# Attention: exponent rows transferred two units sooner, ahead of raw weights, and the row terms' constant operand made in one operation

## The reference

```python
m_new = maximum(f + m, i)
C = exp(f + m - m_new) * C + exp(i - m_new) * outer(v, k)
n = exp(f + m - m_new) * n + exp(i - m_new) * k
y = sigmoid(o) * (C @ q) / maximum(abs(n @ q), 1)
...
x = leaky_relu(x @ w_in) @ w_out                # 1536 x 320, hidden 2048
P = exp(x @ w_gate - max), eight rounds of row and column normalising
out = sum over 8 experts of P[:, e] * (relu(x @ w1[e]) @ w2[e])
```

## Time and profile before

| | |
|---|---|
| median of 3 runs | 940.11 us (940.0 to 940.24) |
| the profiled execution | 939.58 us |
| its span, first to last instruction | 937.9 us |
| PE busy | 928.4 us, 99% |
| VectorE, ScalarE, GpSimd busy | 646.0, 354.1, 436.7 us |
| TensorE clock granted | full in every slice |
| DMA | 42.39 MB, 45 GB/s over the span |

### The profile page before, as it was taken

The page is one execution under the profiler, slowest core; times in us unless marked ns, Lnnn a source line. Parts: engine busy times, 40 slices in busy tenths (PEclk is TensorE's granted clock), DMA queues, the critical chain, the costliest instruction groups (busy, mean ns, idle before and its releaser), DMA issues.

```text
span 937.9 us, 16679 instructions
## 1 busy us (share of the span) xinstructions
PE 928.4 (99%) x6508; PEld 888.6 (95%) x6518; DVE 646.0 (69%) x1071; ACT 354.1 (38%) x671; POOL 436.7 (47%) x489
## 2 busy tenths in 40 slices
PE   9999999999999999999999999999999999999998
PEld 6999888888799999999999999999999999999998
DVE  7877555467778989876666666666666666667665
ACT  6674534344444233233332432333243233323221
POOL 4462311076598645656633651663365166336000
PEclk9999999999999999999999999999999999999999
DMA  7990321011011111021101111111111111110000
GB/s 124 216 146 2 93 64 34 1 35 34 0 38 32 35 35 56 14 59 43 53 17 35 56 47 35 35 38 31 35 50 53 35 35 34 35 35 1 30 28 29
DMA packets 82796, 42.39 MB, mean 45 GB/s; under 512 B 54270, under 2 KB 82302, under 8 KB 82718
## 3 DMA queue, kind: packets, MB, share of 16 engines
q1 hardware_dynamic: 82542, 41.23, 17.2%
q10 hardware_dynamic: 176, 0.10, 0.0%
HBM read 39.13 MB, written 2.11 MB: 44 GB/s over the span
## 4 chain that ended last, share of the span: by engine, by line
PE 88%; DVE 6%; SPq 3%; issue 1%; ACT 1%; DMA 1%; POOL 0%; DVEq 0%; POOLq 0%; ACTq 0%
PE psB L1720 12%; PE psB L1721 11%; PE psB L1722 11%; PE psA L1706 8%; PE psA L1705 8%; PE psA L1704 8%; PE psA L1703 8%; PE psA L1633 8%; PE psB L1652 2%; PE psB L1653 2%; PE psB L1654 2%; PE psA L1513 1%; PE psB L1536 1%; DVE gl L1431 1%; DMA rhs<-parts_d 1%
## 5 line engine op out<-in xcount | busy, mean ns | idle before, releaser
L693 POOL TENSOR_TENSOR wst<-raw_w,wst 128x128 fp32r<-128x128 f32 (+2 forms) x192 | 163.1, 862 | 303.7 <-ACT wst L920 174.9
L1720 PE MATMUL psB<-w2s,gh 128*128 128x320 f32 x768 | 238.6, 311 | 0.9 <-DVE acc L1405 0.9
L1722 PE MATMUL psB<-w2s,gl 128*128 128x320 f32 x768 | 237.3, 309 | 0.0
L1721 PE MATMUL psB<-w2s,gh 128*128 128x320 f32 x768 | 237.3, 309 | 0.0
L1431 DVE SCALAR_TENSOR_TENSOR gl<-part,gh 128x512 fp32r<-128x512 f32 x192 | 160.4, 875 | 63.4 <-ACT gh L1035 62.8
L1035 ACT ACTIVATE gh<-part 128x512 fp32r<-128x512 f32 x192 | 110.7, 624 | 245.2 <-DVE part L1425 245.1
L1705 PE MATMUL psA<-xop,wst 128*128 128x256 f32 x672 | 190.2, 283 | 0.0
L1706 PE MATMUL psA<-xop,wst 96*128 96x256 f32 x672 | 190.2, 283 | 0.0
L1704 PE MATMUL psA<-xop,wst 128*128 128x256 f32 x672 | 190.2, 283 | 0.0
L1703 PE MATMUL psA<-xop,wst 128*128 128x256 f32 x672 | 190.0, 283 | 0.0
L1720 PEld LDWEIGHTS psB<-w2s,gh 128*128 128x128 f32 x768 | 144.6, 188 | 1.4 <-DVE gl L1431 1.1
(11 more groups left out here) (204 smaller groups left out, 1376.8 us busy)
## 6 DMA issues: line engine op xcount, KB each, us to landing
raw_w<-in_moe_w_dram SPq DMA_DIRECT2D x32, 320.0 KB, 3.2
raw_w<-in_moe_w_dram SPq DMA_DIRECT2D x32, 256.0 KB, 2.6
raw_w<-in_moe_w_dram SPq DMA_DIRECT2D x96, 64.0 KB, 2.5
qs<-in_q_dram SPq DMA_DIRECT2D x12, 160.0 KB, 3.4
ks<-in_k_dram SPq DMA_DIRECT2D x12, 160.0 KB, 3.7
vz<-in_v_dram SPq DMA_DIRECT2D x12, 160.0 KB, 4.1
og<-in_o_gate_dram SPq DMA_DIRECT2D x12, 160.0 KB, 4.1
out_dram<-acc SPq DMA_DIRECT2D x5, 320.0 KB, 2.5
```

The source lines that it names most:

```text
L693: return pool.tensor_tensor(dst, raw, high.bitcast(F32), ALU.subtract)
L1720: pe.matmul(bank, gh[:, slot, cols], w2[:, f, 0, :], start=first, stop=False)
L1721: pe.matmul(bank, gh[:, slot, cols], w2[:, f, 1, :], start=False, stop=False)
L1722: last = pe.matmul(bank, gl[:, slot, cols], w2[:, f, 0, :], start=False, stop=end)
```

## The change

Three edits. SyncE: the rows of units 4 and 5 are issued before the output gates and the first raw weights, and inside the loop each step n issues the rows of unit n + 2 behind its own q, k and v. GpSimd: only slot 0 is padded before `cut_row` and `lhs`. VectorE: the eight operations of `fill` become one `tensor_tensor` with both inputs broadcast.

```diff
             load_v(2)
+            for b in range(B):
+                sp.wait_ge(x_done, b + 1)
+                chunk_rows(sp, 2, b)
             load_gates_out(0, range(B, U_IT))
+            load_v(3)
             first_w1(0)
-            load_v(3)
             first_w2(0)
-            for c in range(2, NC):
-
-                for b in range(B):
-                    n = B * c + b
-                    sp.wait_ge(x_done, n - 2 * B + 1)
-                    chunk_rows(sp, c, b)
-                    load_qk(n)
...
+            for n in range(2 * B, NU):
+                load_qk(n)
...
+                load_v(n)
+                if n + B < NU:
+                    sp.wait_ge(x_done, n - B + 1)
+                    chunk_rows(sp, (n + B) // B, n % B)
...
-            for j in range(U_IT):
-                slot_pads(j).then_inc(pads, 1)
+            slot_pads(0).then_inc(pads, 1)
             pool.memset(cut_row[:], 0.0).then_inc(consts, 1)
...
                 pool.tensor_copy(lhs[s][:], cut_row[:].unsqueeze(1).to_broadcast([P, B, L])).then_inc(lhs_ok, 1)
+            for j in range(1, U_IT):
+                slot_pads(j).then_inc(pads, 1)
...
-            fill(0, 0).then_inc(fill_ok, 1)
+            dve.tensor_tensor(rhs[0][:, 0, :, :], at_row[:].unsqueeze(1).to_broadcast([P, H, L]),
+                              head_rows[:].unsqueeze(2).to_broadcast([P, H, L]), ALU.add).then_inc(fill_ok, 1)
```

More of the change, by code:

```diff
@@ L544, in _ @@
             load_v(2)
+            for b in range(B):
+                sp.wait_ge(x_done, b + 1)
+                chunk_rows(sp, 2, b)
             load_gates_out(0, range(B, U_IT))
+            load_v(3)
             first_w1(0)
-            load_v(3)
             first_w2(0)
-            for c in range(2, NC):
-                for b in range(B):
-                    n = B * c + b
-                    sp.wait_ge(x_done, n - 2 * B + 1)
-                    chunk_rows(sp, c, b)
-                    load_qk(n)
[L556 to L566, removed]
+            for n in range(2 * B, NU):
+                load_qk(n)
+                if n == U_IT:
+                    load_gates_out(1)
+                if n == 2 * U_IT - 1:
+                    load_gates_out(2)
+                load_v(n)
+                if n + B < NU:
+                    sp.wait_ge(x_done, n - B + 1)
+                    chunk_rows(sp, (n + B) // B, n % B)
+                if n == U_IT + 1:
+                    first_w1(1)
+                if n == U_IT + 2:
+                    first_w2(1)
+                if n == U_IT + 3:
+                    first_w1(KT)
             for a in range(KT):
```

## The result

The changed kernel takes 942.63 us in the median of 13 executions (941.8 to 947.86); the kernel before, beside it, 940.22 (938.59 to 941.31, 13). The ratio of the two is 1.0047 [1.0034, 1.006]. It is slower, and the median lies 1.4 us above my range. The executions of after fall into two groups: seven between 941.8 and 942.63, with a mean granted clock of 1.0 (0.998 in the profiled one), and six between 945.64 and 947.86, with 0.994 to 0.996. There are two losses to explain: some 2 to 3 us in every execution (2.8 between the profiled ones), and 3 to 6 more in half of them. The profiled execution (942.4 us, span 940.7) is of the first group; its span is 2.8 longer than before's 937.9.

The account below looks back on a forecast made before the run. PE, busy 99% of the span, was taken as the bound. Removing 2.03 us of row waits, mostly offset by later q and k, gave -0.3 us against 940.11: forecast 939.8 us, range 938.4 to 941.2.

Parts of the forecast that it names:

- The rows: PE's waits for row loads at the exponents of units 4 and 8 both go, 2.03 us.
- the sum: PE's arrivals and k waits at units 4, 5, 8; the end moves by s - 1.03, not below -2.03 us.
- Unit 8: At its transposes the 0.70 us row wait goes, k lands at 58.47, PE waits 0.79; 0.13 us is left.
- s: Delay of each q and k load in SyncE's queue behind one more pair of rows: taken as 0.9 us.
- The bound of 2.4 for s: Upper end of the q and k delay: two row pairs issued near 20 us with nothing behind making it up.
- The other bound, -0.4: Lower end of the q and k delay, if 1.3 us of L513's 2.09 us issue dissolves.
- Rival B: Transposes of units 4, 5, 8: q and k delay outgrows the rows' gain; +1.4 us, 941.5; chance 0.12.
- Rival C: Prologue: fill and scan shut out GpSimd, first transposes 0.8 us late; 940.0, or 939.1 with small s; chance 0.11.
- The fill: VectorE's prologue: one operation of 1.3 us replaces eight taking 2.31; worth nothing on PE, 0.3 us on SyncE.
- Raw weights: ScalarE's cast of the third piece at 43.34 may start 0.4 us late; 0 to 0.1 us counted.
- A (q and k in time): Transposes: no wait for q and k, both row waits simply gone; -1.8 us, 938.3; chance 0.14.
- D (rows not sooner): Exponents of units 4 and 8: rows land no sooner, only s is left; +0.9 us, 941.0; chance 0.03.

Follow-up runs that it names:

- rows_only: Kernel before with SyncE's new queue order alone, fill and padding as before: 943.32 us, ratio 1.0041.
- after_again: The changed kernel unaltered, timed and profiled once more: 943.19 us, ratio 1.0045.
- no_fill: Changed kernel with the old fill in eight operations; SyncE's and GpSimd's edits stay: 941.73 us, ratio 1.0037.
- late_fill: Changed kernel, but VectorE's single fill waits until GpSimd has padded slot 0: 946.7 us, ratio 1.0062.
- kept_busy: rows_only plus eleven blank warm-up matmuls on PE in front of unit 8's transposes: 942.02 us, ratio 1.0021.
- late_w1: rows_only with 512 KB of raw weights (L515, L516) moved behind unit 8's q, k and v: 939.65 us, ratio 1.0003.
- spread_gates: rows_only with output gates of units 4 to 11 loaded one unit per step behind v, not four at once: 938.55 us, ratio 0.9989.
- held_k: spread_gates with unit 8's q and k loads held until PE has done unit 8's exponents: 942.4 us, ratio 1.0036.
- spread_after: Changed kernel (single fill, new memset order) with output gates loaded one unit per step: 939.15 us, ratio 0.9996.
- spread_one: spread_after with one small VectorE memset more behind the single fill: 938.53 us, ratio 0.9981.
- spread_seven: spread_after with seven small VectorE memsets behind the single fill: 938.6 us, ratio 0.9983.
- fill_only: Kernel before with the fill in one operation alone, SyncE and padding as before: 940.8 us, ratio 1.0011.
- spread_after_2: spread_after unaltered, timed and profiled once more: 939.7 us, ratio 0.9993.
- fill_warm: fill_only with ten warm-up matmuls instead of eight before PE's first transposes: 940.77 us, ratio 1.001.

## Why the prediction was wrong

- **The rows.** Right. Both waits went. At units 4 and 5 the sum is best checked with rows_only, where PE isn't late: PE arrives at 31.79 and 39.04 and waits 0.46 and 0.53 (31.78, 38.77, 0.78 and 0.33 said). But k's delay there was not made as I had it: unit 4's k was issued sooner than before, not later, and was longer on its way.
- **"Unit 8", and in it the size of s: the step that failed.** The formula (the end moves by s - 1.03) held, as it must where PE waits for that k: it landed at 60.57 instead of 57.57, which makes s 3.0, and s - 1.03 is 1.97 against the measured 2.02. I had put s at 0.9, from the sentence "Everything else ahead of them is the same, so each is issued 1.21 us later if the queue keeps its pace", and I left the 3.8 us from issue to landing as it was. In the profile of after the issue was nearly as said (1.16 later), and the way became 5.64 us: the raw weights in front were moved by 3.46 us and not by 1.2. In the other profiles with this queue both parts were off: the issue was 2.05 us later in after_again, 2.2 in rows_only, 2.9 in no_fill and 3.3 in late_fill, with the four gates ahead holding SyncE for 5.0 to 6.4 us (4.35 before), and in after_again the v behind them for 2.09 (0.83 before); and the way took 4.6 to 4.9. That makes s 2.8 to 4.3. The profile of kept_busy, with the same queue, had 0.5 and 0.9, an s of 1.4 only: it differs much from execution to execution. So neither did the queue keep its pace, nor did the landing follow the issue. late_w1 and spread_gates show what stands behind it: with the 512 KB behind k, or the four gates spread, k of unit 8 is in time.
- **The bound of 2.4 for s** was too low for the same reason. It summed idle stretches of the DMA engines near 20 us, and not what happens to a transfer when a large one ahead of it comes nearer. The other bound, -0.4, had a true ground: L513's issue took 0.66 us instead of 2.09, and k of unit 4 was issued sooner for it. It landed no sooner. Rival B (k outgrows the gain) is what happened. I had its mechanism, but with its place at unit 4 (0.95 late there, "0.1 more at unit 8"), where the loss that counts came from unit 8.
- **What an idle time of PE costs.** The prediction counted it at its length. In all four profiles in which PE was idle for 1.93 us or more at unit 8 (held_k 1.93, rows_only 2.46, no_fill 2.62, late_fill 2.63) it went on at half the granted clock for 6 to 10 us, which costs 3 to 5 us. After 1.78 us (after_again), and after the 1.33 and 0.70 us of before, it did not. About half of the executions of these kernels are in the upper group, with a mean granted clock of 0.994 to 0.996; only the profiled ones show where it fell. That the upper group of after's executions is this same loss is therefore argued from rows_only and no_fill, since the profiled execution of after is of the lower group. The range had no such case. The Trainium skill ("TensorE: Matmul & The Clock Gate", section "Part 1: The HAM clock gate (the "warmup" mystery)") says that the gate's default is the throttled state and that activity releases it. The trace of rows_only agrees: 0.50 granted from 62 us on, after the idle time, rising again in the stretch from 71 us (0.82), with PE busy all the while.
- **Rival C** was right in each step. GpSimd was shut out by the fill and the scan (next rows), the first transposes came 0.64 us late (0.8 said), and the delay disappeared in the waits behind. It took nothing from the end, since k of unit 8 came later still. Where the waits for k are gone, it can: the profiled execution of spread_after, with warm-ups of 3.81 us, is 1.31 us behind spread_gates at unit 8 (58.91 against 57.60).

```profile
2.06 1.22 DVE L1122 TENSOR_TENSOR rhs<-at_row,head_rows 128x1024 bf16<-128x1024 f32 x1 [0.29 <-POOL head_rows L599]
3.50 1.75 DVE L1131 TENSOR_TENSOR_SCAN m_row<-gf,gi 16x768 f32<-16x768 f32 x1 [0.21 <-DMA gf<-in_f_gate_dram]
```

```profile
2.33 1.11 POOL L599 TENSOR_SCALAR_AFFINE_SELECT ident<-ident 128x128 f32<-128x128 f32 x1
...
3.55 2.06 POOL L599 TENSOR_SCALAR_AFFINE_SELECT head_mask<-head_mask 128x3 f32<-128x3 f32 x2
```

- **The fill.** 1.22 us against 1.3 said. In the trace of before the two selects above took 0.37 and 0.53 us. SyncE no longer waits for `parts0`, as said. That fewer instructions of VectorE cost 0.6 us at 329 us was in no part of the prediction; spread_one and spread_seven show it.
- **Raw weights.** ScalarE's third piece was cast at 45.48, right behind the cast of `x` as before, so its lateness is PE's own; nothing to pay.
- **A (q and k in time)** needed s near -0.4; out. **D (rows not sooner)**: out, since the wait went.

Left open: why the clock fell at 37 us in the first profile of after, where PE had been idle only 0.24 and 0.20 us shortly before (after_again didn't show it; a mean clock of 0.998, which such a short fall gives, is also that of many executions of before); whether the upper half of the executions are those in which k came latest; and why the nine warm-ups ran at half rate for a part. They were slow in the four profiles with 0.68 to 0.73 us idle before the first transposes (after, fill_only, spread_after, spread_after_2) and at full rate after 0.64 us and less (spread_one, after_again, fill_warm). That they were slow is read from their durations; the granted clock in the rows is 1.00 there. Why VectorE is idle at one place of its list was not tried further.

## What to carry to other kernels

Where a load is late in a busy queue, work out its landing and not only its issue: ask which large transfers ahead of it move nearer, and how long the issues in front of it hold the queue. When a wait is taken away, the next load behind it is the bound; here the loads had to be spread (one unit's gates per step) before the reordering gave anything. And an idle time of 2 us on TensorE should be priced above its length, since the clock may fall after it.

## What the runs showed of the hardware

- A single VectorE operation with two inputs in SBUF held one GpSimd select of 0.37 us up to 1.11, and the scan held two of 0.53 us up to 2.06. Both ended 0.2 to 0.4 us after VectorE's operation (3.44 behind 3.28, 5.61 behind 5.25), so GpSimd seems to get next to nothing while it runs.
- One VectorE instruction more at 2 us decides whether VectorE is idle for 0.46 us near 318 us (after; 0.45 to 0.47 in all six profiles that have it), and by this whether it comes ahead of a GpSimd operation of 1.6 to 2.0 us or behind it. An operation that takes 0.79 us ahead of it takes 1.62 behind it, and PE waits 0.60 us. A change in the number of instructions is a change of its own.
- PE idle for 1.93 to 2.63 us at full load was followed by half the granted clock for 6 to 10 us in four profiles of four; 1.78 us was not, in one.
- 160 KB in pieces of 160 bytes took 3.3 us from issue to landing with 512 KB behind them (late_w1), 4.6 to 5.6 with the 512 KB just ahead (after, after_again, rows_only). Four such loads in a row held the issuing queue for 4.35 to 6.36 us (before, rows_only).
